# One full-array transpose placed in front of the loop of a convolution and two-layer MLP kernel that runs TensorE as two half-row streams

## The reference, cut to what matters

```python
w = softmax(weight_gen, axis=-1)                 # [2, 4096, 8 heads, 7 taps]
out = np.einsum('bshk,bskhg->bshg', w, x_unf)    # 7 shifted copies of x, 24 features a head
x1 = out.reshape(8192, 192)
h1 = np.maximum(x1 @ w_in1, 0.0);  x2 = (h1 * h1) @ w_out1
h2 = x2 @ w_in2;  y = (h2 * np.clip(h2 + 3.0, 0.0, 6.0) / 6.0) @ w_out2
```

## Time and profile before

| | |
|---|---|
| median of 3 runs | 1168.07 us (1165.64 to 1168.88) |
| the profiled execution's own time | 1168.12 us |
| its span | 1166.3 us |
| TensorE busy | 1153.4 us, 99% |
| VectorE, ScalarE, GpSimd busy | 924.5, 675.9 and 3.7 us |
| mean granted TensorE clock | 1.000 |

### The profile page before, as it was taken

How to read it: one execution, slowest core, us unless ns; L and a number is a source line. 1 busy time by engine, 2 the same in 40 slices (tenths; PEclk the granted TensorE clock), 3 DMA queues, 4 the chain that set the end, 5 groups by cost and what they waited for, 6 DMA issues and landing times.

```text
span 1166.3 us, 26723 instructions
## 1 busy us (share of the span) xinstructions
PE 1153.4 (99%) x10412; PEld 1147.6 (98%) x10412; DVE 924.5 (79%) x1054; ACT 675.9 (58%) x772; POOL 3.7 (0%) x11
## 2 busy tenths in 40 slices
PE   7999999999999999999999999999999999999998
PEld 7999999999999999999999999999999999999997
DVE  8889797887968879697786978879688796976565
ACT  6887645556555565645556455564555556555554
POOL 1000000000000000000000000000000000000000
PEclk9999999999999999999999999999999999999999
DMA  7211003020030200202011020200302002010001
GB/s 214 79 63 53 5 2 76 4 66 12 0 74 4 70 9 13 61 4 72 6 49 29 0 74 4 65 14 0 74 4 69 10 13 61 0 38 3 1 15 28
DMA packets 78190, 41.93 MB, mean 36 GB/s; under 512 B 55952, under 2 KB 72462, under 8 KB 78156
## 3 DMA queue, kind: packets, MB, share of 16 engines
q1 hardware_dynamic: 78156, 41.45, 13.8%
HBM read 30.00 MB, written 11.40 MB: 36 GB/s over the span
## 4 chain that ended last, share of the span: by engine, by line
PE 94%; ACT 2%; DVE 1%; DMA 1%; issue 1%; SPq 0%; DVEq 0%; ACTq 0%
PE h_ps L910 45%; PE y_ps L921 30%; PE y_ps L930 20%; DMA stage<-in_moe_w_in_dram 1%; ACT hid L444 1%; ACT hid L449 1%; ACT win L431 0%; ACT hid_hi L457 0%; DVE acc L610 0%; DVE hid_lo L711 0%; SPq L292 0%; DVE prod L632 0%; DVE wout L677 0%; DVE hid L700 0%; SPq L302 0%
## 5 line engine op out<-in xcount | busy, mean ns | idle before, releaser
L910 PE MATMUL h_ps<-xt,win 64*128 64x512 f32 (+1 forms) x4860 | 1068.9, 379 | 1.0 <-DVE wout L677 0.9
L910 PEld LDWEIGHTS h_ps<-xt,win 64*128 64x128 f32 x4860 | 826.6, 184 | 2.0 <-DVE wout L677 1.3
L921 PE MATMUL y_ps<-hid_hi,wout 64*128 64x512 f32 (+1 forms) x2160 | 562.5, 379 | 0.7 <-DVE win L677 0.5
L460 ACT ACTIVATE hid_hi<-hid 128x1024 fp32r<-128x1024 f32 (+1 forms) x244 | 256.4, 1051 | 316.8 <-DVE hid L702 155.5
L711 DVE TENSOR_TENSOR hid_lo<-hid,hid_hi 128x1024 fp32r<-128x1024 f32 (+1 forms) x270 | 313.2, 1160 | 143.0 <-ACT hid_hi L460 137.8
L921 PEld LDWEIGHTS y_ps<-hid_hi,wout 64*128 64x128 f32 x2160 | 385.2, 184 | 1.9 <-DVE win L677 0.7
L921 PE MATMUL y_ps<-hid_lo,wout 64*128 64x512 f32 (+1 forms) x1080 | 323.1, 378 | 1.0 <-DVE hid_lo L711 1.0
L930 PE MATMUL y_ps<-hid_lo,wout 64*128 64x512 f32 (+1 forms) x1080 | 322.9, 378 | 0.0
L930 PE MATMUL y_ps<-hid_hi,wout 64*128 64x512 f32 (+1 forms) x1080 | 322.8, 378 | 0.0
L921 PEld LDWEIGHTS y_ps<-hid_lo,wout 64*128 64x128 f32 x1080 | 194.6, 184 | 1.7 <-DVE hid_lo L711 1.4
L930 PEld LDWEIGHTS y_ps<-hid_hi,wout 64*128 64x128 f32 x1080 | 194.6, 184 | 0.2
(11 more groups left out here) (87 smaller groups left out, 325.8 us busy)
## 6 DMA issues: line engine op xcount, KB each, us to landing
xwin<-in_x_dram SPq DMA_DIRECT2D x14, 960.0 KB
by_feature<-stage SPq DMA_DIRECT2D x52, 96.0 KB, 2.0
out_dram<-outs SPq DMA_DIRECT2D x240, 16.0 KB, 1.5
out_dram<-outs SPq DMA_DIRECT2D x240, 8.0 KB, 1.4
stage<-by_feature SPq DMA_DIRECT2D x13, 256.0 KB, 3.0
stage<-in_moe_w_out_dram SPq DMA_DIRECT2D x8, 384.0 KB, 5.8
stage<-in_moe_w_in_dram SPq DMA_DIRECT2D x4, 512.0 KB, 6.9
stage<-in_moe_w_in_dram SPq DMA_DIRECT2D x8, 256.0 KB, 6.2
```

Of the source, the lines that this page charges most:

```text
L460: act.activation(hi, hid[:, slot, :, 0:width], ACT.Copy).then_inc(hi_done, 1)
L910: return pe.matmul(h_ps[:, s % 2, t, 0:tokens.stop - tokens.start], win[layer][r, wn, cols], src[r, xn, tokens], start=bool(rows) and n in ...
L921: return pe.matmul(ps[:, 0, tokens], wout[layer][r, tile, w_cols], src, start=bool(rows) and s == 0 and n == 0, stop=not rows and s == STE ...
```

## The change

A function `together` is added and called once, at step 39 (`ALONE - 1`), between `head` and `first_body`. It waits as `sums_free` does and then issues one transpose of the 128x128 identity on all 128 rows, with its result in the first 128 columns of the PSUM slot of step 39. Nothing reads the result; the hidden sums of the step overwrite it with their first matmul.

```diff
+            def together(g):
+
+                sums_free(g, True)
+                pe.transpose(h_ps[:, g % 2, 0, 0:P], ident[:, :], ident[:, :])
+
...
                 inn = (layer, s, xt[int(layer == 0 and g >= 2 * STEPS) ^ 1], half)
+                if g == ALONE - 1:
+                    together(g)
                 first_body(g, inn, late, g >= HALVES + 2)
```

## The result

Twenty runs of each kernel have medians of 1168.52 us before and 1165.33 us after. One run of after, 1252.02 us at a mean granted clock of 0.85, and one of before beside the experiments, 1615.17 us at 0.655, are left out of everything that follows; without the first the median of after is 1165.26 us. The ratio of the means is 0.9977 with a 95% interval of 0.9970 to 0.9984, so that the mean is 2.7 us lower: a small change, but the interval leaves out 1. The forecast was 1168.8 us, 0.7 us slower.

A forecast was written before the change was run, and what follows sets the result against it. TensorE, busy 99% without waits in the loop, was taken as the bound, its issue rate unchanged. 1168.12 us + 0.74 us for the drain = 1168.86 us, less 0.05 us for the median: 1168.8 us, range 1164.0 to 1172.0.

The forecast's parts named there:

- the drain: At step 39, going from half rows to the full array and back delays the lower stream once by 0.74 us.
- the full clock in the loop: At the loop's start, the transpose's possible effect on the granted clock was put at nothing.
- 0.18 us less cover: In the loop, the closest `hid_lo` delivery's cover falls from 0.93 us to 0.75 us; no wait appears.
- the lasting alignment: Late in the loop both streams still start together; aligned through the loop at the same rate had chance 0.72.
- a change of rate in the loop: From step 40 on, the streams' offset costs nothing, so a step stays at 4.433 us.
- the 15 ns that it had named as the sign of being wrong: In the loop, a step differing from 4.433 us by 15 ns or more would prove the prediction wrong.
- the transpose and the exit: At step 39, 0.11 us for the transpose's columns and 0.27 us for returning to half rows.
- the stated range: For the total, 1164.0 to 1172.0 us: drain bounds 1168.4 to 1169.4, widened twice by run spread, 2.4 down, 0.8 up.
- With nobody beside it, at any offset, one stream takes the 0.233 us of a pair.: Behind the last pair, the lone lower stream's 0.2329 us intervals were read as showing that moving a stream gains nothing.
- These steps already do what the change sets up for the loop, and no faster: In the 256-column steps, aligned and offset stretches take 0.1184 and 0.1189 us a pair, differing by at most 0.5%.
- aligned streams run faster on 512 columns: In the loop, aligned half-row streams regain 6.2 ns a matmul, 27.3 us in all, giving 1141.5 us; chance 0.10.

The follow-up runs named there:

- the first bench: Changed kernel plus nine blocks of 512-column pairs at different offsets, then lone-stream and full-array blocks, at step 39; 36 lone matmuls took 8.67 us and 8.63 us.
- The second bench: Changed kernel plus blocks of 256-column pairs behind step 39's transpose, with 0 to 224 extra upper columns; streams took 118.5 to 118.9 ns or 120.0 ns.
- kernel 9: Changed kernel plus 40 blocks of 14 pairs behind step 39's transpose, each starting 0.8 ns later; loop behind them 4.4333 us a step, streams together.
- kernel 10: Changed kernel with a wait replacing the transpose, plus an extra 384-column upper matmul; 4.4152 us a step, streams 0.15 us apart, 8 of 12 runs under 1167 us.
- 3: Changed kernel plus one 384-column upper matmul behind the transpose; 8 of 12 runs at 1164.1 to 1165.6 us, 4 at 1168.2 to 1169.8.
- 4: Changed kernel with the transpose at step 36 instead of 39, so half-row transposes of step 38 follow it; all 11 runs at 1168.7 to 1169.9 us.
- 11: The kernel before, unchanged, traced once more; 1168.20 us and 4.4333 us a step.
- 15: Changed kernel plus an extra 256-column upper matmul behind the transpose; 0 of 12 runs under 1167 us, slow trace.
- Kernel 6: Changed kernel with the transpose replaced by a wait for the last upper matmul at step 39; 1164.6 to 1166.4 us, ratio to before 0.9978.

## Why the prediction was wrong

The place and roughly the size of the drain, the full clock in the loop, the absence of waits in spite of 0.18 us less cover, and the lasting alignment came as forecast. What failed is the term that the prediction put at nothing, a change of rate in the loop: it kept 4.433 us a step, and 4.4152 us were measured. That is 18 ns less, beyond the 15 ns that it had named as the sign of being wrong, and 232 x 0.0181 = 4.2 us in all. Beside it the 0.11 us by which the drain was set too high, nearly all of it in the transpose and the exit, is small. The measured median lies in the stated range, but through no insight: the range was widened by the spread of the runs of before. (Its own widening, 2.4 us down and 0.8 us up, twice, gives 1163.6 to 1171.0 us and not 1164.0 to 1172.0.) The rate term failed at two steps.

"With nobody beside it, at any offset, one stream takes the 0.233 us of a pair. The pair is no slower than one stream, so there is no time between the streams to be won": the reading was right and the conclusion not. The lone stream had 0.233 us because it went on with the cadence of the loop in front of it. After the change the same lone stream takes 231.9 ns over its 8 intervals, and the first bench has lone streams of both kinds. One sample of a rate was taken for its bound.

"These steps already do what the change sets up for the loop, and no faster": the two stretches of 256 columns were different in lag and equal in cadence. To 1 ns both have 118.6 to 118.7 ns a pair. The second bench has 118.9 and 120.0 ns side by side. The tolerance was misjudged as well: 4.52 and 4.50 us from rows to 0.01 us can differ by 0.9%, not 0.5%, and the effect looked for was 0.4%. Even 0.5% of the 232 steps is 5 us, more than the gain.

The rival "aligned streams run faster on 512 columns", with a chance of 0.10, came true in its sign, at 0.9 ns a pair and not 6.2; but its mechanism is not what did it, since aligned streams can be slow (kernel 9) and streams apart fast (kernel 10). What the change does is to replace a start after which 18% of the runs are in the lower group by one after which, for common starts behind an empty array, 84% are (18 of 19 with the change itself). The median steps from one group to the other: the 3.8 us between the groups of before, less the 0.6 us of the drain, are 3.2 us, and the medians differ by 3.3 us (1168.52 and 1165.26). The mean gains 2.7 us, since neither kernel is always in its group.

The three runs of before (1168.88, 1168.07, 1165.64 us) held the hint: they are of both groups, a spread of 3.2 us in a kernel whose TensorE does not wait in its loop. The prediction used it to widen the range and did not ask where it came from.

**Still open.** What makes the two cadences, and what picks one at a start, no run shows; the number of transposes does not order them. That the cadences set the rate is shown, by traces of both kinds with and without alignment; why the start that the change makes picks the fast one so often is not. A mix is as slow as two slow streams (3, 4, 11 and 15), so a start pays only if both pick the fast cadence, but a common moment alone does not see to that: kernel 4 has it, and none of its runs is in the lower group. Nor does an empty array alone: kernel 15 has it, with the upper stream pushed by 256 columns, and has none there either, while 3 and 10, pushed by 384, have 8 of 12 each. The counts were not traced run by run. Kernel 6 and the change can't be told apart (0.9978 and 0.9977), and no kernel here beats both by a measurable amount; of the two, the wait needs no extra instruction on the array.

## What to carry to other kernels

Where one engine is the bound and never waits for another, a rate read from one stretch is a sample, not a limit: look at the intervals between starts, not at their mean, and compare them in several runs. If the runs of an unchanged kernel fall in two groups, explain the groups before costing an edit smaller than their distance, and compare kernels by the share of runs in each. And before giving the credit to the arrangement that an edit makes, build its two opposites: the arrangement with the slow rate, and the fast rate without the arrangement.

## What the runs showed of the hardware

- A stream of weight load and matmul on 64 rows by 512 columns at the full 2.4 GHz (granted clock 1.00) had two stable cadences here, 229 and 238 ns by turns (233.3) and a cycle of 228, 230, 232, 241, 232, 231, 232 (232.4). It kept the one it started with for the 990 us of the loop's 224 steps beside another stream, and for 36 matmuls alone; a full-array stream had the second too.
- With 256 columns a cycle of five (118.6 to 118.9 ns) stands beside cycles of two and three (120.0 ns), 1% apart.
- Of two streams of different cadence the fast one gains 0.9 ns a pair and goes on to be ahead of the other; from step 72 on it is held to the slower rate at 0.18 to 0.41 us ahead (3, 4, 11, 15), and alone again it has its own cadence (11). What holds it was not tried.
- A change from half rows to the full array costs 0.32 us from start to start, the way back 0.26 us with the 128 columns of the transpose in it, and the second matmul of a half-row stream comes 0.11 us later than in the loop.
- The weight loads' busy share tells how far two streams overlap, not how fast they go: 84% aligned and fast (the change), 80% aligned and slow (9), 100% apart at either rate (before, 10).
